# A linear-attention and two-MLP kernel: tree maxima of k, weight split steps moved, last rows stored from ScalarE's queue

## What is computed

```python
q_s = exp(q - max(q, axis=-1)); q_s = q_s / (sum(q_s, axis=-1) + 1e-09)
k_s = exp(k - max(k, axis=2));  k_s = k_s / (sum(k_s, axis=2) + 1e-09)
kv = einsum('bhsd,bhse->bhde', k_s, v)
x = einsum('bhsd,bhde->bhse', q_s, kv)          # then tokens x 512
h = x @ w_in                                     # 512 -> 2048
g = maximum(h, 0) + alpha * minimum(h, 0)
x2 = g @ w_out                                   # 2048 -> 512
h = x2 @ w_in2                                   # 512 -> 1024
solu = h * softmax(h)
out = (layer_norm(solu) * g_ln) @ w_out2         # 1024 -> 512
```

## Time and profile before

| | |
|---|---|
| median of the runs | 1207.49 us |
| profiled execution | 1208.86 us |
| its span | 1207.1 us |
| mean granted clock of TensorE | 0.994 of full speed |
| TensorE busy | 1187.6 us, 98% |
| VectorE busy | 891.2 us, 74% |
| ScalarE busy | 538.2 us, 45% |
| GpSimd busy | 309.1 us, 26% |
| moved by DMA | 225 MB, mean 186 GB/s |

### The profile page before, as it was taken

One profiled execution on the slowest core, in us unless ns is written; L12 is line 12 of the kernel. 1 busy time (PEld: TensorE's weight loads), 2 busy tenths in 40 slices (PEclk: granted clock), 3 DMA queues, 4 the chain that ended last, 5 costly groups with the idle time before them and its releaser, 6 DMA issues.

```text
span 1207.1 us, 16162 instructions
## 1 busy us (share of the span) xinstructions
PE 1187.6 (98%) x6013; PEld 982.4 (81%) x6013; DVE 891.2 (74%) x1165; ACT 538.2 (45%) x744; POOL 309.1 (26%) x233
## 2 busy tenths in 40 slices
PE   7999999999999999999999999999999999999998
PEld 6878887887888888888888888898788888888886
DVE  7768777786775475977769777686898787878772
ACT  4534534434354344443444344443556464545452
POOL 5722414132242000000000000036544535353310
PEclk8999999999999999999999999999999999999999
DMA  9998877869874735264270542498346545454444
GB/s 231 255 259 260 244 254 217 271 202 273 270 237 166 266 133 191 96 205 144 83 239 28 189 159 70 142 290 266 122 149 192 176 134 174 136 177 130 145 153 129
DMA packets 211918, 225.07 MB, mean 186 GB/s; under 512 B 63208, under 2 KB 148224, under 8 KB 211712
## 3 DMA queue, kind: packets, MB, share of 16 engines
q1 hardware_dynamic: 206064, 212.50, 56.4%
q0 software_dynamic: 5728, 11.53, 3.3%
q10 hardware_dynamic: 48, 0.01, 0.0%
HBM read 128.51 MB, written 95.48 MB: 186 GB/s over the span
## 4 chain that ended last, share of the span: by engine, by line
PE 83%; DVE 8%; DMA 4%; issue 2%; SPq 2%; ACT 1%; POOL 0%; ACTq 0%; DVEq 0%
PE ps_y L1965 9%; PE ps_y L1966 9%; PE ps_y L1967 9%; PE ps_y L2051 5%; PE ps_y L2053 5%; PE ps_y L2055 5%; PE ps_y L2109 5%; PE ps_y L2111 5%; PE ps_y L2110 5%; PE ps_m L2053 3%; PE ps_m L2055 3%; PE ps_m L2051 3%; PE ps_m L2090 2%; PE ps_m L2094 2%; PE ps_m L2092 2%
## 5 line engine op out<-in xcount | busy, mean ns | idle before, releaser
L1965 PE MATMUL ps_y<-X,W 128*128 128x512 f32 x576 | 227.2, 394 | 0.0
L1967 PE MATMUL ps_y<-X,W 128*128 128x512 f32 x576 | 224.6, 390 | 0.0
L1966 PE MATMUL ps_y<-X,W 128*128 128x512 f32 x576 | 224.6, 390 | 0.0
L1421 DVE SCALAR_TENSOR_TENSOR gst<-gst,nslope,ps_y 128x512 f32<-128x512 f32 x144 | 104.4, 732 | 113.4 <-ACT gst L993 113.0
L993 ACT ACTIVATE gst<-ps_y 128x512 f32<-128x512 f32 x144 | 85.8, 596 | 225.6 <-PE ps_y L1967 166.4
L854 POOL TENSOR_TENSOR x2r<-x2r 128x256 f32<-128x256 f32 x18 | 25.2, 1401 | 406.9 <-DMA x2r<-x_scratch 406.9
L1965 PEld LDWEIGHTS ps_y<-X,W 128*128 128x128 f32 x576 | 108.4, 188 | 23.5
L1967 PEld LDWEIGHTS ps_y<-X,W 128*128 128x128 f32 x576 | 108.3, 188 | 22.9
L1966 PEld LDWEIGHTS ps_y<-X,W 128*128 128x128 f32 x576 | 108.4, 188 | 21.8
L2051 PE MATMUL ps_y<-rh,WOc 128*128 128x512 f32 (+1 forms) x320 | 117.9, 369 | 1.1 <-DVE rl L1583 1.1
L2053 PE MATMUL ps_y<-rl,WOc 128*128 128x512 f32 (+1 forms) x320 | 117.7, 368 | 0.0
(11 more groups left out here) (189 smaller groups left out, 2534.6 us busy)
## 6 DMA issues: line engine op xcount, KB each, us to landing
g_scratch<-gst SPq DMA_DIRECT2D x144, 256.0 KB, 3.6
RX<-g_scratch SPq DMA_DIRECT2D x36, 512.0 KB, 3.6
z_scratch<-zb SPq DMA_DIRECT2D x36, 512.0 KB, 3.5
zt<-z_scratch SPq DMA_DIRECT2D x144, 128.0 KB, 2.8
ws_scratch<-whl SPq DMA_DIRECT2D x22, 512.0 KB, 4.5
RY<-g_scratch SPq DMA_DIRECT2D x18, 512.0 KB, 4.6
RZ<-g_scratch SPq DMA_DIRECT2D x18, 512.0 KB, 4.7
x2r<-x_scratch SPq DMA_DIRECT2D x18, 512.0 KB, 5.1
```

Source lines behind the costliest of these rows:

```text
L1421: nc.vector.scalar_tensor_tensor(gst[:, n % 3, :], gst[:, n % 3, :], nslope[:, f:f + 1], ps_y[:, f % 4, :], ALU.mult, ALU.add).then_inc(g_ ...
L1965: nc.tensor.matmul(o, W1[:, f, 0, a, :], x[:, 0, a, :], start=(a == 0), stop=False)
L1966: nc.tensor.matmul(o, W1[:, f, 0, a, :], x[:, 1, a, :], start=False, stop=False)
L1967: mm = nc.tensor.matmul(o, W1[:, f, 1, a, :], x[:, 0, a, :], start=False, stop=(a == KT - 1))
```

## The change

Five edits:

1. `k_main`: one strided reduction of 128x1024 to 128x256 becomes a maximum of two halves of the four token quarters (128x512, into kmt, a buffer that `k_blocks` also writes) and a maximum of the two results (128x256). kmain_ok counts four a batch.
2. WS_AT and WS_LOADS: the pieces' steps become 1, 4, 7, 11, and loads 1, 2 and 3 go to (2, 8), (4, 5) and (5, 5).
3. Inside a step: on SP a piece's store goes ahead of the store of g; on ScalarE the order becomes kv_high, ws_high, exponentials of k; on VectorE ws_low and ws_turn go behind the maxima of k.
4. In the head, the first maxima of q go ahead of the copies of the slopes' columns.
5. The last 64 rows are stored by ScalarE's own DMA queue; SP has three DMAs there instead of four.

```diff
--- before.py
+++ after.py
@@ -302,9 +302,9 @@
         SUM_AT = {1: 0, 2: 1, 3: 2, 6: 3}
 
 
-        WS_AT = (1, 6, 10, 13)
+        WS_AT = (1, 4, 7, 11)
         WS_W2, WS = 14, 14 + NF2
-        WS_LOADS = {(0, 15): 0, (2, 11): 1, (4, 7): 2, (5, 7): 3}
+        WS_LOADS = {(0, 15): 0, (2, 8): 1, (4, 5): 2, (5, 5): 3}
         WS_SUMS = (1, 1, 2, 3, 3, 4, 4)
 
         class Piece:
@@ -534,6 +534,8 @@
                 for f in range(NF):
                     if c == 0 and f + 4 < NF:
                         load_w(f + 4)
+                    if ws_piece(c, f - 1) is not None:
+                        store_ws(ws_piece(c, f - 1))
                     if f > 0:
                         store_g(c, f - 1)
                     if c == 0 and 3 <= f <= 7:
@@ -569,8 +571,6 @@
                         store_xr(b)
                     if (c, f) in WS_LOADS:
                         load_ws(WS_LOADS[c, f])
-                    if ws_piece(c, f - 1) is not None:
-                        store_ws(ws_piece(c, f - 1))
                 store_g(c, NF - 1)
                 if b + 1 < B:
                     load_v_part(b + 1, TT)
@@ -682,7 +682,7 @@
                 u, r = pair_at(n)
                 sp.wait_ge(o_ok, 2 * n + t + 1)
                 if u == PAIRS:
-                    for i in range(2):
+                    for i in range(1 if 2 * n + t == TILES - 1 else 2):
                         b = 2 * (2 * t + r) + i
                         sp.dma_start(out[b * S + TOK:(b + 1) * S, :], ost[i * REM:(i + 1) * REM, t, :]).then_inc(o_st[t], 16)
                 else:
@@ -1047,13 +1047,13 @@
                         q_exp(b, 1)
                     if f == (4 if c == 0 else 3):
                         q_exp(b, 2)
+                    if f == 11:
+                        kv_high(b)
+                    if ws_piece(c, f) is not None:
+                        ws_high(ws_piece(c, f))
                     if f == 7:
                         for piece in range(3):
                             k_exp(b, piece)
-                    if ws_piece(c, f) is not None:
-                        ws_high(ws_piece(c, f))
-                    if f == 11:
-                        kv_high(b)
                     if f == 12:
                         qr_copy(b)
                     if f == (13 if c == 0 else 12):
@@ -1288,6 +1288,8 @@
             out_copy(16, 1)
             out_copy(17, 0)
             out_copy(17, 1)
+            act.wait_ge(o_ok, TILES)
+            act.dma_start(out[B * S - REM:B * S, :], ost[REM:P, 1, :]).then_inc(o_st[1], 16)
 
 
         @block.vector
@@ -1296,13 +1298,21 @@
                 dve.wait_ge(k_in[b % 2][n + 1], 16 * (b // 2 + 1))
                 if b > 0:
                     dve.wait_ge(kt_done, min(b, 2))
-                nc.vector.tensor_reduce(kmax[:, n * HH * D:(n + 1) * HH * D].rearrange("p (h d) -> p h d", h=HH),
-                                        main(K[b % 2])[:, n * HH:(n + 1) * HH, :, :].rearrange("p h t d -> p h d t"),
-                                        AX_X, ALU.max).then_inc(kmain_ok, 1)
+                if b > 2:
+                    dve.wait_ge(kx_ok, b - 2)
+                part = main(K[b % 2])[:, n * HH:(n + 1) * HH, :, :]
+                tops = kmt[:, :].rearrange("p (h t d) -> p h t d", h=HH, t=2)
+                count = 4 * b + 2 * n
+                if count > 0:
+                    dve.wait_ge(kmain_ok, count)
+                nc.vector.tensor_tensor(tops, part[:, :, 0:2, :], part[:, :, 2:4, :], ALU.max).then_inc(kmain_ok, 1)
+                dve.wait_ge(kmain_ok, count + 1)
+                nc.vector.tensor_tensor(kmax[:, n * HH * D:(n + 1) * HH * D].rearrange("p (h d) -> p h d", h=HH),
+                                        tops[:, :, 0, :], tops[:, :, 1, :], ALU.max).then_inc(kmain_ok, 1)
 
             def k_rem(b):
                 dve.wait_ge(k_in[b % 2][0], 16 * (b // 2 + 1))
-                dve.wait_ge(kmain_ok, 2 * (b + 1))
+                dve.wait_ge(kmain_ok, 4 * (b + 1))
                 nc.vector.tensor_tensor(kmax[0:REM, :], kmax[0:REM, :], flat(K[b % 2], 0), ALU.max).then_inc(kmax_ok, 1)
 
             def k_max(b):
@@ -1473,11 +1483,11 @@
                     nc.vector.tensor_tensor(s, A12, s, ALU.subtract).then_inc(wo_sum, 1)
 
             k_max(0)
+            q_max(0, 0)
             dve.wait_ge(at_done, 1)
             nc.vector.tensor_copy(acols[:, :], ps_h[:, 1, 0:NF + NF2]).then_inc(acols_ok, 1)
             dve.wait_ge(acols_ok, 1)
             nc.vector.tensor_scalar(nslope[:, :], slope, -1.0, 1.0, ALU.mult, ALU.add).then_inc(acols_ok, 1)
-            q_max(0, 0)
             k_columns(0)
             q_max(0, 1)
             q_max(0, 2)
@@ -1540,9 +1550,6 @@
                         kv_norm(b)
                     if f == 11:
                         kv_low(b)
-                    if ws_piece(c, f) is not None:
-                        ws_low(ws_piece(c, f))
-                        ws_turn(ws_piece(c, f))
                     if c == 0 and f == 13:
                         q_low_second(0)
                         q_low_second(1)
@@ -1554,6 +1561,9 @@
                             k_rem(b + 1)
                         if f == 11:
                             k_blocks(b + 1)
+                    if ws_piece(c, f) is not None:
+                        ws_low(ws_piece(c, f))
+                        ws_turn(ws_piece(c, f))
                     if f == 14:
                         x_low(b, 0)
                         x_low(b, 1)
```

## The result

The changed kernel takes 1220.31 us (median of four, 1217.51 to 1220.77) against 1207.34 for the kernel before in the same comparison (four, 1205.42 to 1207.53): ratio 1.0106, 95% interval 1.0088 to 1.0125. It is slower by 13 us, outside the range of 1202.5 to 1214.0. Two executions in this document's comparisons ran much longer at a lower granted clock (1983.85 us, one of e7_head_as_before and the profiled one, and 1317.08, one of the kernel before), and the times given leave them out. The changed kernel's profiled execution took 1220.77 us with a span of 1219.0, 11.9 more than the span before.

What follows compares the result with a forecast made beforehand. TensorE, busy 98%, was taken as the bound, the memory queue second. Terms 0 - 0.6 - 2.1 + 3.7 + 1.1 + 0.5 = +2.6 us on the 1207.49 median gave 1210.1 us, range 1202.5 to 1214.0.

Steps and rivals of the forecast that it cites:

- Direction and main step: Slower, because ws_high, waiting for the early load, holds ScalarE's exponentials of k and so TensorE's kv product; chance 50%.
- Pass 4: Load 2 holds the exponentials: kv product wait 2.5, clock fall 2.1, old kvf wait gone -0.85; +3.7 us.
- Pass 5: Same order for load 3, K's data earlier, wait 1.3 less 0.2, no clock fall: +1.1 us, bounds -0.2 and +2.2.
- Pass 2: Earlier load 1 cures the x product's waits and clock fall (-4.0); new xr product wait +1.9: -2.1 us.
- Pass 1: Piece's store ahead of g, step 4's store meeting K's data: +0.5 us, bounds 0 to +0.8.
- The clock: TensorE at 1.2 GHz behind idle time: 1.7 us lost in old pass 2; 2.1 with issue gaps added in pass 4.
- Maxima of k: Pairs of maxima give VectorE 6 to 12 us back; worth 0 in loop and head, head bounds -1.5 and 0.
- the sign against V: Batch 0's kv product starting by 16.4 would show V was not the head's limit; 1 us more off.
- Last rows: At the end, one of SP's four stores moves to ScalarE's queue: -0.6 us, bounds -0.6 and 0.
- The lock between VectorE and GpSimd: If GpSimd starts first, ws_low(13) takes 2.0 instead of 0.8; passes 4 and 5 each wait 1.2 more: +2.4 us.
- rival B: Clock also falls in passes 2 and 5 (about 2 each, 10%), or GpSimd first (+2.4, 5%): 1212.5 to 1214; 15%.
- The range: Whole-kernel time, leaving out the half of the load-in-time case below 1202.5 and the worse case's upper end.

Runs made afterwards that it cites:

- e7_head_as_before: e3 with batch 0's maxima by the strided reduction and the first maxima of q where they stood: 1208.07 us, ratio 1.0003.
- e2: Changed kernel with a piece's store on SP back at the end of the step, behind the store of g: 1215.91 us, ratio 1.0071.
- e1: Changed kernel with ScalarE's exponentials of k ahead of ws_high again: 1215.19 us, ratio 1.0065.
- e3: Changed kernel with the weight pieces' steps, loads and orders as before; tree maxima, head order and last rows kept: 1209.47 us, ratio 1.002.
- e10: e3 with 40 filling matmuls ahead of batch 0's kv product in place of 24: 1208.7 us, ratio 1.001.
- e4: Changed kernel with loads 2 and 3 one step later, at (4, 6) and (5, 6): 1220.66 us, ratio 1.0116.
- e8: Changed kernel with exponentials ahead of ws_high and store of g ahead of the piece's store, new steps kept: 1205.84 us, ratio 0.9988.
- e6: Kernel before with only the weight pieces' new schedule (steps, loads, orders on SP, ScalarE and VectorE): 1219.48 us, ratio 1.01.
- e11: e8 with the head as before, as in e7_head_as_before: 1206.81 us, ratio 0.9994.

## Why the prediction was wrong, point by point

*Direction and main step.* Right: slower, by the load in front of the exponentials. In pass 4 the sum holds closely. The load was taken to land at 268.2 and the exponentials to be ready at 270.5; ws_high started when it landed, at 268.85, and the kv product at 271.10. The pass itself began 1.0 us later than before, so within it the landing came 0.35 us earlier than forecast, and the wait was 2.1 us (forecast 2.5). Pass 4 was priced at +3.7 and measured +4.2. That it comes so close is partly luck: the wait was 0.4 less than priced and the fall of the clock cost 0.8 more.

*Pass 5: the term that failed most.* Priced +1.1, measured +5.7. The step that failed: K's data is through up to 2.2 us earlier against the kv product, so the wait is 1.2 us shorter than in pass 4, without a fall of the clock. The wait was 2.9, longer than in pass 4, and the clock fell for 6.8 us (3.0). The load in pass 5, and ScalarE behind it:

```profile
318.02 0.46 SPq L468 DMA_DIRECT2D wst<-w_out_dram  x1
...
326.15 0.72 ACT L1004 ACTIVATE whl<-wst,acols 128x512 fp32r<-128x512 f32 x1 [4.42 <-DMA wst<-w_out_dram]
```

K's head start was indeed smaller here: its loads went out at 309.60, behind the piece's store that now holds SP ahead of g, and TensorE came to the kv product at 325.5, 15.9 us later and not the 17.2 of the earlier trace rows. But that isn't what decided. e2 has the full 17.2 and waits 2.6 all the same, and load 3 took 8.1 us from its issue to its landing in both. What sets the wait is the load's own issue: 17.0 us into the pass (16.1 in pass 4) and 8.1 to landing (8.3), which makes the wait 0.8 longer than in pass 4. The piece's store came only 0.2 later in the pass; the rest is SP's issue of the store of g ahead of the load, 1.23 us instead of 0.47, and why it took that long is open. e1 takes the wait away (57.4 to 53.8), e2 doesn't.

*Pass 2.* Priced -2.1, measured 0, the second largest miss. The new wait was rightly placed, at the xr product behind ScalarE's late negative(11), kv_high, ws_high and qr_copy, and was 2.44 for 1.9. What failed is that it was priced without a fall of the clock, which was kept as a bound (+0.4). By the rows then at hand, 1.9 idle had been enough for one; a wait of 1.9 should have been priced with it (e1's pass 2, with a wait of 2.0 and no fall, shows that it need not come). e2 shows the other part: with g ahead of the piece's store the wait is 0.4 and pass 2 takes 51.97. And the 4.0 that the prediction took off came from one profile; e3 and e10 lose 1.0 and 1.6 in pass 2 with the same schedule.

*Pass 1.* Priced +0.5, bounds to +0.8; measured +1.7. Right mechanism, mis-sized: it was priced by step 4's store meeting K's data, and SP's wait for the piece of step 1, and so for load 0 (3.12 us on ScalarE), was not counted.

*The clock.* Its cost was taken from the one fall of pass 2, 1.7 us. The falls behind the exponentials lasted 6.8 us and cost about 3.0 each. The prediction's own rows had such a one: it calls the fall in the head "the same", but the earlier trace rows have 6.8 us there, behind 2.8 of idle time, and 3.4 in pass 2.

*Maxima of k.* Right in the loop: VectorE's pair took 0.73 + 0.55 against 1.96, 11.0 us less in all (forecast 6 to 12), and no pass of the changed kernel is shorter for it; whether it had a part in the shorter pass 2 of e3 and e10 is open. In the head, "0, bounds -1.5 and 0" held in the changed kernel's profile (kv product at 17.27 against 17.51), but for another reason than V: where TensorE waited longer there, in e2, e4 and e8 (3.2, 1.1 and 2.1 us), it was for the exponentials of k, and in e4 the product started at 16.38, which the prediction had named as the sign against V. And the bound left out the other side: e2's head was 3.6 us longer.

*Last rows.* -0.6 priced; the time from TensorE's last instruction to the end of the span went from 5.24 to 4.74, -0.5. e6, without this edit, has 5.23, and all other profiled runs have 4.73 to 4.76.

*The lock between VectorE and GpSimd*, rival B's second part: didn't come at the place that was priced. VectorE was first and ws_low(13) took 0.63 us; no run here has it the other way round there. It came at another, which the prediction left out: in passes 1 and 2 the ws_low of step 11 started 0.3 us behind GpSimd's qTl (124.38 and 180.24) and took 1.56 and 1.55 us, against 0.7 for the other twelve of that line. SP's store of that piece goes out only then (126.24 and 182.09), ahead of g and of the last part of QN. No wait of TensorE over 0.3 us hangs on it in the changed kernel.

*The range.* Falls of the clock in passes 2 and 5 were kept as an extra of rival B, at 10% and about 2 us each, on top of small waits. Both came, and with longer waits, at 1.6 and 3.0 us. Both terms have the same step wrong, idle time priced without the slower clock behind it. The falls don't all hang on one order, either: e1 takes away those of passes 2, 4 and 5, e2 those of 2 and 4. Of the 9.3 us between the forecast's +2.6 and the +11.9 of the spans, pass 5 is 4.6, pass 2 2.1, pass 1 1.2 and pass 4 0.5; another 0.8 is the difference between the 1.5 behind the passes and the 0.7 given back ahead of them, and 0.1 the end.

## What to carry to other kernels

Where a schedule moves loads earlier, look at what stands behind each new wait on every engine that issues in order: an early load is worth something only if its user is not put ahead of what the busiest engine needs, and a store that waits for another engine should be the last thing of its step on a shared queue, not the first. Price idle time of TensorE with the slower clock behind it. And part a change like this before dropping it: two orders made the whole loss of 13 us, and with them undone, the head as before and one piece moved, nearly the same steps gave a kernel 1.6 us faster than before.

## What the runs showed of the hardware that I had not expected

- A wait of 2.1 us at TensorE was followed by 6.8 us at 1.2 GHz in the changed kernel (pass 4), one of 2.4 us by 3.4 (pass 2), one of 3.1 (e6_ws_alone, pass 5) by 10.2, and one of 2.0 (e1_exp_first, pass 2) and one of 2.1 (e8_exp_and_g_first, head) by none. So the length of a fall can't be read off the wait alone. Its price by the busy time of the pass was 1.6 us (changed kernel, pass 2) to 4.7 (e6_ws_alone, pass 5).
- In one profile (e2's head) earlier work made real work slower: filling matmuls done at 2.4 GHz ran out sooner than at 1.2, and the clock fell in the real work behind the wait.
- A step later in the program is not a step later in time: in e4 the loads moved by a step and went out 0.9 and 0.5 us later, because SP stood at a store's wait in front of them either way.
- What remains open: why single executions of kernels with the same code in a stretch differ by 2 to 3 us there (pass 0 from 53.5 to 56.6, pass 2 from 52.5 to 55.5 with the schedule of before, the stages behind the passes from 717.8 to 720.7), and what made e11's run of 1212.4. No experiment parted these.
